# One attention and MoE kernel: where the next chunk's scores, k's transposition and the decays stand in the steady slots

## The chip, the cores and the metric

The kernel runs on one core of one Trainium2 chip. The metric is the device time of one execution in microseconds (us). The version before the change takes 626.73 us, the median of three executions (626.13 to 627.73).

## What is computed

Three stages follow each other, for 4 batches of 768 tokens with 384 channels (8 heads of 48). All arithmetic is fp32; a dense product is made of three products of a rounded part ("hi") and a rest ("lo").

```python
for t in range(S):                                   # stage 1
    state = alpha[:, :, t, :, None] * state + np.einsum('bhd,bhe->bhde', k[:, :, t], v[:, :, t])
    y[:, :, t] = np.einsum('bhd,bhde->bhe', q[:, :, t], state)
...
theta = x @ w_theta                                  # stage 2
zr = x * cos_t
zi = x * sin_t
y = w_tok_r @ zr + w_tok_i @ zi                      # mixes tokens
u = x + y
x2 = u + np.maximum(u @ w_ch, 0.0)
...
h = np.maximum(x2 @ w_in, 0.0)                       # stage 3: gate with a spatial mix
u, v = (h[..., :d_ff // 2], h[..., d_ff // 2:])
v_s = np.einsum('ts,bsd->btd', w_spatial, v_n) + b_spatial[None, :, None]
out = (u * v_s) @ w_out
```

## The kernel before

Stage 1 is done in chunks of 128 tokens: 6 chunks a batch, 24 in all (`ALL`), numbered g. Within a chunk the recurrence is turned into products: the decays are scanned (`decay_keys`, L738 and L742, and `decay_queries`, L747, on VectorE), keys and queries are multiplied by them (`scale_keys` L931, `scale_queries` L935, on GpSimd), the scores k times q are made on TensorE (`scores` L342), masked on VectorE (`mask_scores` L753), and multiplied by v, with the carried state's share added (`attend`, L370 and L375). The state is carried with a transposition of k (`turn_k` L332), its copy on ScalarE (`copy_kT` L552), the product with v (`keys_values` L354) and `update_state` (L769, L773) on VectorE. Each chunk's result x goes on at once to stage 2: copied (`copy_x` L557), transposed (`transpose_x` L382), split (`xT_high` L562, `xT_low` L780), kept (`keep_xT` L568), multiplied by w_theta (`angles` L391), reduced and put through sine and cosine (`whole_turns` L575 and L578, `reduce_angle` L786 to L792, `sines` L584 to L587), multiplied (`multiply_z` L797) and split again (`z_high` L598, `z_low` L948).

The program has a slot for each chunk. In the first six slots the kernel fills up. The 18 slots behind them, g = 6 to 23, are the steady ones: beside chunk g's stage 1 they hold stage 2 of the batch before. A steady slot has two units of `token_mix` (L409, 18 matmuls each; `ya` and `yb` in the code) and one tile of `channel_mix` (L428). A unit is one chunk of one half of a batch; six units fill the accumulator psY, and then `make_u` (L808, three instructions on VectorE) adds x and empties it. That is so in the slots with c = g % 6 equal to 0 and 3. The first unit of the next half follows in the next slot, and each third of it waits for its `make_u` (`u_made`). `make_x2` (L815) finishes a channel tile.

All engines run orders written out by hand, with semaphores between them; each executes its own list in that order. SyncE issues the transfers, in order too. `load_chunk(g)` brings decays, keys and queries of chunk g (L254, 770 KB, tile `akq`) and v (L255) into one of two buffers, and so waits until `attend(g-2)` has read the old contents. `store_x2` (L264) waits for `make_x2`, and stands in front of the load of chunk 2 of a batch (from the second steady batch on) and of that of chunk 5:

```python
for c in range(CHUNKS):
    load_chunk((b + 1) * CHUNKS + c)
    if c == 1 and b:
        store_x2(b - 1, 1)
    if c == 4:
        store_x2(b, 0)
```

The buffers of the partial sums in PSUM are psS (scores), psF (in two halves: psK for k's transposition and the state's product, psO for attention and x's transposition), psY and psC. Stage 3, behind the slots, is not touched by the change.

Of the kernel before, what the change touches and what calls it, by code (L numbers as in the profile page):

```python
# [24 lines left out]
CHUNKS = SEQ // P  # L25
# [11 lines left out]
ALL = BATCH * CHUNKS  # L37
LINKS = CHUNKS - 1
# [37 lines left out]
def build(nc, akq, v_in, w_theta, w_tok_rT, w_tok_iT, w_ch, w_in, w_spT, b_sp, w_out, out, x2_dram):  # L76
    ctx = ExitStack()
    with ctx:
# [246 lines left out]
        def _(pe):  # L325
            def turn_k(g):
                if g % CHUNKS == LINKS:
                    return
                pe.wait_ge(k_scaled, g + 1)
                need(pe, state_made, link(g))  # L330
                for p in range(PAIRS):
                    mm = pe.transpose(psK[:, tile(p)], K[g % 2][:, p, :], ident[:])  # L332
                mm.then_inc(kT_made, 1)

            def scores(g):
                s = g % 2
                pe.wait_ge(q_scaled, g + 1)
                need(pe, masked, g)
                for p in range(PAIRS):
                    for h in range(2):  # L340
                        rows = slice(64 * h, 64 * h + HD)
                        mm = pe.matmul(psS[:, h, p, :], K[s][rows, p, :], Q[s][rows, p, :],  # L342
                                       start=True, stop=True)
                mm.then_inc(scored, 1)
# [13 lines left out]
            def attend(g):  # L358
                s, c = g % 2, g % CHUNKS
                pe.wait_ge(v_arrived[s], 16 * (g // 2 + 1))  # L360
                pe.wait_ge(masked, g + 1)
                need(pe, xT_lo, g)
                need(pe, xT_kept, g)
                if c:
                    pe.wait_ge(state_made, link(g))
                for p in range(PAIRS):
                    for h in range(2):
                        e = slice(HD * (2 * p + h), HD * (2 * p + h + 1))
                        for rows in TOKEN_HALVES:
                            mm = pe.matmul(psO[rows, e], probs[:, h, p, rows], V[s][:, e],  # L370
                                           start=(p == 0 and h == 0), stop=False, skip_group_check=True)
                    if c:
                        pr = slice(2 * HD * p, 2 * HD * (p + 1))
                        for rows in TOKEN_HALVES:
                            mm = pe.matmul(psO[rows, pr], Q[s][:, p, rows], S[c % 2][:, p, :],  # L375
                                           start=False, stop=(p == PAIRS - 1), skip_group_check=True)
                mm.then_inc(attended, 1)

            def transpose_x(g):
                pe.wait_ge(x_copied, g + 1)  # L380
                for j in range(CT):
                    mm = pe.transpose(psO[:, tile(j)], x[g % 2][:, tile(j)], ident[:])  # L382
                mm.then_inc(xT_made, 1)
# [11 lines left out]
            def token_mix(unit):  # L395
                if unit is None:
                    return
                k, s = unit
                h = k % HALVES
                if k < HALVES:  # L400
                    pe.wait_ge(tok_lo, k * CHUNKS + s // 2 * 2 + 2)
                if h == 0:
                    pe.wait_ge(z_lo, k // HALVES * CHUNKS + s + 1)
                for j in range(CT):
                    if s == 0:
                        need(pe, u_made, (k - 1) * CT + j + 1)
                    for q, W in enumerate((WR, WI)):
                        for n, (l, m) in enumerate(PASSES):
                            mm = pe.matmul(psY[:, j, 0:HALF], Z[s][l][:, q, tile(j)], W[m][:, s, half(h)],  # L409
                                           start=(s == 0 and q == 0 and n == 0),  # L410
                                           stop=(s == CHUNKS - 1 and q == 1 and n == 2))
                    if s == CHUNKS - 1:
                        mm.then_inc(y_made, 1)
                if s < CHUNKS - 1:
                    mm.then_inc(mixed, 1)
# [17 lines left out]
            for c in range(CHUNKS):  # L433
                ya, yb = units(-1, c)
                turn_k(c)
                scores(c)
                if c == 1:
                    pe.wait_ge(theta_lo, 1)
                if c:
                    angles(c - 1, 0)  # L440
                token_mix(ya)
                keys_values(c)
                attend(c)
                transpose_x(c)
                token_mix(yb)
            angles(CHUNKS - 1, 0)
            for b in range(BATCH - 1):
                for c in range(CHUNKS):
                    g = (b + 1) * CHUNKS + c
                    ya, yb = units(b, c)  # L450
                    n = tile_of(b, c)
                    turn_k(g)
                    scores(g)
                    token_mix(ya)
                    keys_values(g)
                    attend(g)
                    channel_mix(n, g)
                    transpose_x(g)
                    token_mix(yb)
                    angles(g, 0 if n is None else n + 1)  # L460

# [51 lines left out]
            b = BATCH - 1  # L513
# [32 lines left out]
        def _(act):  # L546
            def copy_kT(g):
                if g % CHUNKS == LINKS:
                    return
                act.wait_ge(kT_made, link(g) + 1)  # L550
                need(act, kv_made, link(g))
                act.activation(kT[:].rearrange("p q d -> p (q d)"), psK, ACT.Copy).then_inc(kT_copied, 1)  # L552
# [75 lines left out]
            for c in range(CHUNKS):  # L628
# [13 lines left out]
                for i in SPLITS[c]:  # L642
                    tok_high(i)

            for b in range(BATCH - 1):
                for c in range(CHUNKS):
                    g = (b + 1) * CHUNKS + c
                    whole_turns(g - 1)
                    copy_kT(g)
                    if c == 1:  # L650
                        u_highs(HALVES * b)
                    if c == 4:
                        u_highs(HALVES * b + 1)
                    sines(g - 1)
                    z_high(g - 1)
                    copy_x(g)
                    xT_high(g)
                    keep_xT(g)
                    for i in SPLITS[g]:
                        tok_high(i)  # L660

# [66 lines left out]
        def _(dve):  # L728
# [93 lines left out]
            for c in range(CHUNKS):  # L822
                mask_scores(c)
                decay_keys(c + 1)
                if c:
                    reduce_angle(c - 1)
                decay_queries(c + 1)
                update_state(c)
                xT_low(c)
                if c:  # L830
                    multiply_z(c - 1)
            for b in range(BATCH - 1):
                for c in range(CHUNKS):
                    g = (b + 1) * CHUNKS + c
                    reduce_angle(g - 1)
                    mask_scores(g)
                    multiply_z(g - 1)
                    if g + 1 < ALL:
                        decay_keys(g + 1)
                        decay_queries(g + 1)  # L840
                    xT_low(g)
                    make_x2(tile_of(b, c))
                    update_state(g)
                    if c == 0:
                        make_u(HALVES * b)
                    if c == 3:
                        make_u(HALVES * b + 1)
# [79 lines left out]
        def _(pool):  # L927
# [42 lines left out]
            for c in range(CHUNKS):  # L970
                scale_keys(c + 1)
                scale_queries(c + 1)
                if c:
                    z_low(c - 1)
                if c == CHUNKS - 2:
                    pool.wait_ge(ch_hi, 1)
                    pool.tensor_tensor(WC[1][:], raw_ch[:], f(WC[0][:]), ALU.subtract).then_inc(ch_lo, 1)
                for i in SPLITS[c]:
                    tok_low(i)
            for b in range(BATCH - 1):  # L980
                for c in range(CHUNKS):
                    g = (b + 1) * CHUNKS + c
                    if c == 1:
                        u_lows(HALVES * b)
                    if c == 4:
                        u_lows(HALVES * b + 1)
                    z_low(g - 1)
                    if g + 1 < ALL:
                        scale_keys(g + 1)
                        scale_queries(g + 1)  # L990
                    for i in SPLITS[g]:
                        tok_low(i)
            z_low(ALL - 1)
# [68 lines left out]
```

## Time and profile before

| | |
|---|---|
| median of three executions | 626.73 us |
| the profiled execution: its own time | 626.28 us |
| the profiled execution: its span | 624.6 us |
| mean granted TensorE clock, share of full | 0.986 |
| TensorE busy with matmuls | 591.7 us, 95% |
| VectorE busy | 363.1 us, 58% |
| ScalarE busy | 224.0 us, 36% |
| GpSimd busy | 257.7 us, 41% |
| steady slots in the span | from about 81 us to 326 us |

The span is the time from the first to the last recorded instruction. A line such as `L409 PE MATMUL psY<-tok_r_hi,z_hi` names the line of the kernel, the engine (PE is TensorE's matmuls, PEld its weight loads, DVE VectorE, ACT ScalarE, POOL GpSimd, SPq the transfers that SyncE issues), the operation, and what it writes and reads. A float32 matmul counts twice in the profile, so that `scores`, 8 instructions in the program, appears as x16. In the chain of work that ended last, the start of a piece is the end of the piece before it.

### The profile page before, as it was taken

The page shows a single profiled execution, that of the slowest core. Times are in us where ns is not written, and L with a number is a line of the kernel's source. Part 1 is how long each engine was busy: PE and PEld are TensorE (multiplying, and loading weights), DVE is VectorE, ACT ScalarE, POOL GpSimd, SP SyncE. Part 2 cuts the span into 40 slices and gives each one's busy share as a digit, 9 for nine tenths or more (in the row PEclk, how much of TensorE's full clock was granted, in tenths as well). Part 3 has the DMA queues.
Part 4 walks back from the last instruction along what each step waited for, and adds up shares of the span by engine and source line. Part 5 has one row for each costly group of instructions (what it writes and reads, how often), then busy time and mean ns, then how long its engine had stood idle before and what let it go on. Part 6 is the DMA issues. An engine that isn't in the chain of part 4 may idle for free.

```text
span 624.6 us, 11166 instructions
## 1 busy us (share of the span) xinstructions
PE 591.7 (95%) x4608; PEld 560.6 (90%) x4608; DVE 363.1 (58%) x565; ACT 224.0 (36%) x410; POOL 257.7 (41%) x205
## 2 busy tenths in 40 slices
PE   4778989999999999999997999999999999999998
PEld 3667889999999999999996978998999899989997
DVE  5788666787786776877734037846333633373132
ACT  2544556343343444433434114623131313131210
POOL 5475578353463353644513017245313531352130
PEclk9978999999999999999998999999999999999999
DMA  8551321132141231320323073010220020002002
GB/s 314 203 178 65 111 82 64 64 102 66 65 165 65 61 106 65 105 95 32 102 102 114 0 266 114 8 70 2 76 77 2 0 77 1 0 1 77 0 2 77
DMA packets 20259, 49.54 MB, mean 79 GB/s; under 512 B 1648, under 2 KB 15216, under 8 KB 19696
## 3 DMA queue, kind: packets, MB, share of 16 engines
q1 hardware_dynamic: 20208, 48.81, 22.8%
q8 instruction: 37, 0.61, 0.4%
q14 instruction: 14, 0.11, 0.1%
HBM read 39.37 MB, written 9.44 MB: 78 GB/s over the span
## 4 chain that ended last, share of the span: by engine, by line
PE 86%; DVE 5%; ACT 3%; POOL 3%; issue 2%; DMA 0%; DVEq 0%; ACTq 0%; POOLq 0%
PE psY L409 22%; PE psF L508 8%; PE psS L508 8%; PE psC L391 7%; PE psC L428 7%; PE psS L486 5%; PE psS L342 5%; PE psF L476 5%; PE psF L486 3%; PE psS L496 3%; PE psF L496 3%; PE psF L370 3%; PE psS L476 3%; PE psF L375 2%; PE psF L332 2%
## 5 line engine op out<-in xcount | busy, mean ns | idle before, releaser
L948 POOL TENSOR_TENSOR z_lo<-cos_sin,z_hi 128x768 fp32r<-128x768 f32 x24 | 44.0, 1833 | 125.6 <-ACT z_hi L598 125.6
L1012 POOL TENSOR_TENSOR gated_lo<-u_gated,gated_hi 128x384 fp32r<-128x384 f32 x32 | 32.4, 1013 | 125.4 <-ACT gated_hi L698 125.3
L409 PE MATMUL psY<-tok_r_hi,z_hi 128*128 128x384 f32 x144 | 52.5, 365 | 4.7 <-POOL z_lo L948 4.3
L747 DVE TENSOR_TENSOR_SCAN akq<-akq,rtotal 128x516 f32<-128x516 f32 x24 | 54.7, 2281 | 0.7
L409 PE MATMUL psY<-tok_r_hi,z_lo 128*128 128x384 f32 x144 | 48.5, 337 | 0.0
L409 PE MATMUL psY<-tok_r_lo,z_hi 128*128 128x384 f32 x144 | 48.5, 337 | 0.0
L409 PE MATMUL psY<-tok_i_lo,z_hi 128*128 128x384 f32 x144 | 48.4, 336 | 0.0
L409 PE MATMUL psY<-tok_i_hi,z_lo 128*128 128x384 f32 x144 | 48.4, 336 | 0.0
L409 PE MATMUL psY<-tok_i_hi,z_hi 128*128 128x384 f32 x144 | 48.4, 336 | 0.0
L931 POOL TENSOR_TENSOR akq<-akq,after 128x512 f32<-128x512 f32 x24 | 44.7, 1862 | 4.9 <-DVE after L738 4.9
L698 ACT ACTIVATE gated_hi<-u_gated 128x384 fp32r<-128x384 f32 x32 | 16.8, 526 | 81.0 <-DVE u_gated L886 81.0
L955 POOL TENSOR_TENSOR u_lo<-u_f,u_hi 128x384 fp32r<-128x384 f32 x24 | 24.4, 1046 | 50.2 <-ACT u_hi L603 50.2
L786 DVE SCALAR_TENSOR_TENSOR psC<-turns,psC 128x384 f32<-128x384 f32 x24 | 13.5, 562 | 53.3 <-ACT turns L578 53.2
L370 PE MATMUL psF<-v,scores 128*64 128x48 f32 x768 | 36.7, 223 | 0.5 <-DVE scores L753 0.5
L738 DVE TENSOR_TENSOR_SCAN after<-akq,restart 128x516 f32<-128x516 f32 x24 | 33.7, 1403 | 3.6 <-DMA akq<-akq 3.6
L753 DVE TENSOR_TENSOR scores<-psS,mask 128x1024 f32<-128x1024 f32 x24 | 29.2, 1217 | 11.2 <-PE psS L342 11.2
L1006 POOL TENSOR_TENSOR vn_lo<-vt,vn_hi 128x512 fp32r<-128x512 f32 x24 | 31.2, 1305 | 8.4 <-ACT vn_hi L683 8.4
L409 PEld LDWEIGHTS psY<-tok_r_hi,z_hi 128*128 128x128 f32 x144 | 27.3, 189 | 7.7 <-POOL z_lo L948 3.6
L575 ACT ACTIVATE turns<-psC 128x384 f32<-128x384 f32 x24 | 11.8, 490 | 62.0 <-PE psC L391 62.0
L370 PEld LDWEIGHTS psF<-v,scores 128*64 128x64 f32 x768 | 31.8, 141 | 1.6 <-issue 1.6
L508 PE MATMUL psF<-sp_hi,vn_hi 128*128 128x384 f32 x96 | 32.2, 335 | 0.8 <-DVE sp_lo L913 0.8
L935 POOL TENSOR_TENSOR akq<-akq 128x512 f32<-128x512 f32 x24 | 28.5, 1186 | 10.4 <-DVE akq L747 10.4
(141 smaller groups left out, 1747.3 us busy)
## 6 DMA issues: line engine op xcount, KB each, us to landing
akq<-akq SPq DMA_DIRECT2D x23, 770.0 KB, 4.5
v<-v_in SPq DMA_DIRECT2D x24, 192.0 KB, 4.7
x_dram<-u_f SPq DMA_DIRECT2D x8, 576.0 KB, 3.7
x_raw<-x_dram SPq DMA_DIRECT2D x4, 1152.0 KB, 5.5
out<-ot SPq DMA_DIRECT2D x24, 192.0 KB, 1.9
raw_tok_r<-w_tok_rT SPq DMA_DIRECT2D x6, 384.0 KB, 7.8
raw_tok_i<-w_tok_iT SPq DMA_DIRECT2D x6, 384.0 KB, 8.7
raw_sp<-w_spT SPq DMA_DIRECT2D x1, 2304.0 KB, 8.9
```

The costliest lines, as they stand in the source:

```text
L370: mm = pe.matmul(psO[rows, e], probs[:, h, p, rows], V[s][:, e], start=(p == 0 and h == 0), stop=False, skip_group_check=True)
L391: mm = pe.matmul(psC[:, 0:D], XT[g % 2][l][:, j, :], WT[m][:, j, :], start=(j == 0 and k == 0), stop=(j == CT - 1 and k == 2))
L409: mm = pe.matmul(psY[:, j, 0:HALF], Z[s][l][:, q, tile(j)], W[m][:, s, half(h)], start=(s == 0 and q == 0 and n == 0), stop=(s == CHUNKS - ...
L428: mm = pe.matmul(psC[:, 0:HALF], WC[l][:, j, tile(m_out)], U[m][:, j, :], start=(j == 0 and k == 0), stop=(j == CT - 1 and k == 2))
L476: mm = pe.matmul(banks[n % RING], X2[l][:, j, tile(i)], WN[m][:, j, G:FF], start=(j == 0 and k == 0), stop=(j == CT - 1 and k == 2))
L486: mm = pe.matmul(banks[n % RING][:, 0:D], GA[l][:, j, tile(i)], WO[m][:, j, :], start=(j == 0 and k == 0), stop=(j == GT - 1 and k == 2))
L496: mm = pe.matmul(banks[n % RING][:, 0:HALF], WN[l][:, j, tile(j_out)], X2[m][:, j, half(h)], start=(j == 0 and k == 0), stop=(j == CT - 1 ...
L508: mm = pe.matmul(banks[n % RING][:, 0:HALF], VN[l][:, s, tile(j)], WS[m][:, s, half(h)], start=(s == 0 and k == 0), stop=(s == CHUNKS - 1 ...
L738: dve.tensor_tensor_scan(after[:, ::-1], ALPHA[s][:, ::-1], restart[:, ::-1], 1.0, ALU.mult, ALU.add).then_inc(after_made, 1)
L747: dve.tensor_tensor_scan(ALPHA[s], ALPHA[s], rtotal[:, 1:], rtotal[:, 0:1], ALU.mult, ALU.add).then_inc(decayed, 1)
L931: pool.tensor_tensor(K[g % 2], K[g % 2], AFTER[:, :, 1:SEG], ALU.mult).then_inc(k_scaled, 1)
L948: pool.tensor_tensor(Z[c][1][:], trigs[g % 2][:], f(Z[c][0][:]), ALU.subtract).then_inc(z_lo, 1)
```

## The change

In the steady slots TensorE makes the scores of chunk g+1 right behind the attention of chunk g, where those of chunk g stood at the head of the slot, and transposes k of chunk g+1 right behind x of chunk g. The first two (for g = 6) are put into the last filling slot. On VectorE the state's update and the mask of chunk g+1 come earlier, and the decays, now those of chunk g+2, stand behind `xT_low` and ahead of `make_u`; decays for chunk 7 stand ahead of the steady slots. GpSimd scales chunk g+2, and ScalarE copies k's transposition at the end of a slot. SyncE's list stays.

```diff
 # TensorE
                 attend(c)
+                if c == LINKS:
+                    scores(CHUNKS)
                 transpose_x(c)
+                if c == LINKS:
+                    turn_k(CHUNKS)
                 token_mix(yb)
...
-                    turn_k(g)
-                    scores(g)
                     token_mix(ya)
                     keys_values(g)
                     attend(g)
+                    if g + 1 < ALL:
+                        scores(g + 1)
                     channel_mix(n, g)
                     transpose_x(g)
+                    if g + 1 < ALL:
+                        turn_k(g + 1)
                     token_mix(yb)
 # ScalarE
+            copy_kT(CHUNKS)
...
                     whole_turns(g - 1)
-                    copy_kT(g)
...
                     keep_xT(g)
+                    if g + 1 < ALL:
+                        copy_kT(g + 1)
 # VectorE
+            mask_scores(CHUNKS)
+            decay_keys(CHUNKS + 1)
+            decay_queries(CHUNKS + 1)
...
                     reduce_angle(g - 1)
-                    mask_scores(g)
                     multiply_z(g - 1)
+                    update_state(g)
                     if g + 1 < ALL:
-                        decay_keys(g + 1)
-                        decay_queries(g + 1)
+                        mask_scores(g + 1)
+                    make_x2(tile_of(b, c))
                     xT_low(g)
-                    make_x2(tile_of(b, c))
-                    update_state(g)
+                    if g + 2 < ALL:
+                        decay_keys(g + 2)
+                        decay_queries(g + 2)
                     if c == 0:
                         make_u(HALVES * b)
                     if c == 3:
                         make_u(HALVES * b + 1)
 # GpSimd
+            scale_keys(CHUNKS + 1)
+            scale_queries(CHUNKS + 1)
...
                     z_low(g - 1)
-                    if g + 1 < ALL:
-                        scale_keys(g + 1)
-                        scale_queries(g + 1)
+                    if g + 2 < ALL:
+                        scale_keys(g + 2)
+                        scale_queries(g + 2)
                     for i in SPLITS[g]:
                         tok_low(i)
```

How the rows move is shown at two places. The first is VectorE's list in slot g = 9 (c = 3 of the first steady batch). The scans are printed under the operation they are built from; L738 and L747 are the two of the decays, u_f_0_82<-psC is `make_x2`, and u_f_1_83<-psY is `make_u`. Before:

```order
L753 TENSOR_TENSOR scores<-psS,mask 128x1024
L797 TENSOR_TENSOR cos_sin_97<-x_73,cos_sin_97 128x768
L738 SCALAR_TENSOR_TENSOR after<-akq_86,restart 128x516
L742 RECIPROCAL rtotal<-after 128x4
L747 SCALAR_TENSOR_TENSOR akq_86<-akq_86,rtotal 128x516
L780 TENSOR_TENSOR xT_lo<-psF,xT_hi 128x384
L815 SCALAR_TENSOR_TENSOR u_f_0_82<-psC,u_f_0_82 128x384
L769 TENSOR_TENSOR psF<-psF,state_94 64x192 x2
L773 TENSOR_TENSOR state_93<-psF,after 64x4x48 x2
L808 TENSOR_TENSOR u_f_1_83<-psY,xT_kept_80 128x384 x3
```

And after the change, with new line numbers (each is 8 higher):

```order
L805 TENSOR_TENSOR cos_sin_97<-x_73,cos_sin_97 128x768
L777 TENSOR_TENSOR psF<-psF,state_94 64x192 x2
L781 TENSOR_TENSOR state_93<-psF,after 64x4x48 x2
L761 TENSOR_TENSOR scores<-psS,mask 128x1024
L823 SCALAR_TENSOR_TENSOR u_f_0_82<-psC,u_f_0_82 128x384
L788 TENSOR_TENSOR xT_lo<-psF,xT_hi 128x384
L746 SCALAR_TENSOR_TENSOR after<-akq_87,restart 128x516
L750 RECIPROCAL rtotal<-after 128x4
L755 SCALAR_TENSOR_TENSOR akq_87<-akq_87,rtotal 128x516
L816 TENSOR_TENSOR u_f_1_83<-psY,xT_kept_80 128x384 x3
```

The decays moved from ahead of `xT_low` to the place directly in front of `make_u`, and they read the other buffer, akq_87: that of chunk 11, which slot 9's own attention (chunk 9) has to leave first.

The second place is TensorE's list from chunk 6 on, in the last filling slot, as the difference between the two programs:

```order
 L370 MATMUL psF<-v_90,scores 64x48 x4
 L375 MATMUL psF<-state_94,akq_87 64x96 x2
+L342 MATMUL psS<-akq_86 128x128 x8
 L382 MATMUL psF<-ident,x_74 128x128 x3
-L409 MATMUL psY<-tok_r_hi,z_hi 128x384
...
 L332 MATMUL psF<-ident,akq_86 128x128 x4
-L342 MATMUL psS<-akq_86 128x128 x8
+L409 MATMUL psY<-tok_r_hi,z_hi 128x384
```

Scores stand behind attention now, and k's transposition behind that of x; the token mix and the angles follow. In the steady slots the two go the same way, one slot ahead of their chunk.

## Rows read from the trace of the kernel before

**Rows 1.** Waits of TensorE over the span: waited for, us, times, longest

```profile
PE psY L409 <- POOL z_lo L948: 4.3, 2, 3.3
...
PE psY L409 <- DVE u_f L808: 0.4, 1, 0.4
```

**Rows 2.** Chain of waits, slot 15: start us, us, what

```profile
203.80 1.09 PE psS L342 x16
204.89 3.35 PE psY L409 x18
208.24 0.60 PE psF L354 x16
...
210.45 1.78 PE psC L428 x9
...
212.56 3.12 PE psY L409 x18
215.68 1.56 PE psC L391 x9
...
218.77 3.34 PE psY L409 x18
```

**Rows 3.** Timeline of VectorE, slot 15: start us, us, what

```profile
208.46 1.23 DVE L738 TENSOR_TENSOR_SCAN after<-akq,restart 128x516 f32<-128x516 f32 x1
...
209.94 2.48 DVE L747 TENSOR_TENSOR_SCAN akq<-akq,rtotal 128x516 f32<-128x516 f32 x1
...
213.59 0.55 DVE L815 SCALAR_TENSOR_TENSOR u_f<-psC,u_f 128x384 f32<-128x384 f32 x1
...
215.59 1.49 DVE L808 TENSOR_TENSOR u_f<-psY,xT_kept 128x384 f32<-128x384 f32 x3
```

**Rows 4.** Timeline of the transfers that SyncE issues, slots 15 and 16

```profile
214.17 0.53 SPq L264 DMA_DIRECT2D x_dram<-u_f  x1
214.74 0.62 SPq L254 DMA_DIRECT2D akq<-akq  x1
```

**Rows 5.** Landing of loads L254: that of slot 15, of slot 18, then the page, all 23

```profile
L254 SPq DMA_DIRECT2D akq<-akq x1: 617/617/617, 214.7 to 214.7; - x1
DMA to landing us min/median/max: 5.7/5.7/5.7
L254 SPq DMA_DIRECT2D akq<-akq x1: 617/617/617, 254.8 to 254.8; - x1
DMA to landing us min/median/max: 6.6/6.6/6.6
...
akq<-akq SPq DMA_DIRECT2D x23, 770.0 KB, 4.5
```

**Rows 6.** Timeline, VectorE scan L747 in the second filling slot

```profile
13.89 2.10 DVE L747 TENSOR_TENSOR_SCAN akq<-akq,rtotal 128x516 f32<-128x516 f32 x1
```

**Rows 7.** Timeline of GpSimd at the same place: keys scaled

```profile
13.72 1.18 POOL L931 TENSOR_TENSOR akq<-akq,after 128x512 f32<-128x512 f32 x1 [1.17 <-DVE after L738]
```

**Rows 8.** Chain of waits, slot 18 (c = 0)

```profile
250.49 1.76 PE psC L428 x9
...
258.80 3.35 PE psY L409 x18
```

**Rows 9.** Windows: us, busy PE, PEld, DVE, ACT, POOL, PEclk, DMA share, GB/s

```profile
36.80:40.70 3.90, 0.00 (x0) 0.00 (x0) 3.81 (x7) 1.82 (x4) 2.54 (x3) 0.88 0.62 238
40.80:46.50 5.70, 5.70 (x28) 5.15 (x29) 3.86 (x4) 2.55 (x4) 3.44 (x2) 0.50 0.00 0
...
330.50:333.70 3.20, 0.00 (x0) 0.00 (x0) 0.90 (x2) 0.84 (x1) 1.80 (x1) 0.93 0.55 141
333.70:336.60 2.90, 2.86 (x9) 2.86 (x10) 1.73 (x2) 2.82 (x3) 0.00 (x0) 0.50 0.94 290
```

**Rows 10.** Timeline of GpSimd before the first steady slot

```profile
75.49 1.20 POOL L935 TENSOR_TENSOR akq<-akq 128x512 f32<-128x512 f32 x1 [1.17 <-DVE akq L747]
```

**Rows 11.** Timeline of TensorE at the same place: transposition of x of chunk 5

```profile
75.25 0.44 PE L382 MATMUL psF<-ident,x 128*128 128x128 f32 x2 [0.59 <-ACT x L557]
```

## The prediction

> **What bounds the kernel now.** I read four views in this order. First the waits of TensorE: in the steady slots almost nothing is there. A token mix waited for `z_low` twice, 4.3 us in all, and for `make_u` once, 0.4 us [rows 1]. So in these slots the span is TensorE's own work, one instruction behind another, and the chain of waits says the same: in slot 15 each piece is TensorE's, and from one first token mix to the next it takes 218.77 - 204.89 = 13.88 us [rows 2]. Whatever the other engines do there is hidden as long as it comes in time. Second, the same chain prices the order of TensorE's pieces. Third, VectorE's timeline shows what its list holds in front of `make_u`, which the next half's token mix needs. Fourth, the transfers: where in SyncE's list the loads stand and when they land.
>
> **TensorE's own pieces.** Nothing is added or taken away, only moved. Eighteen matmuls of the token mix take 3.12 us when they follow other full-size matmuls, and 3.35 when they follow the scores, whose operands have 48 rows [rows 2]. Nine take 1.56 us as angles and 1.78 as the channel tile behind attention, whose outputs have 64 columns. So it costs about 0.2 us to come to full size from a small form. Before, a slot pays that twice, behind the scores and behind attention; after, scores follow attention directly, and full size is entered once. The token mix gets back 3.35 - 3.12 = 0.23 us. The scores' own entry stays in their 1.09 us if it costs the same from attention as from a transposition. No row shows that entry. It could be free, or cost two entries; by 0.2 us either way the gain of a slot is 0 to 0.45. I take 0.23, since both known entries are that size. The Trainium skill (TensorEngine Tiling (Array Packing), Key Properties) states that a change of the tiling mode drains the engine, and not a change of tile within one. No run here shows attention followed by scores. By that rule every slot has three changes instead of four, and the gain is one entry a slot, as I take it. From the first token mix of slot 7 to that of slot 23 there are 16 slots: **-3.7 us** (0 to -7).
>
> **The decays, and what they stand in front of.** `decay_keys(g+2)` in slot g needs the load of chunk g+2. That goes into the buffer that `attend(g)` reads, so it cannot start before slot g's attention has ended. In a plain slot this is in time: the median load lands 4.5 us after issue [rows 5], about when `xT_low` is through, and VectorE's next work is due only when the angles end.
>
> In five slots it isn't: g = 9, 12, 15, 18 and 21. There SyncE's list has a `store_x2` in front of the load, which waits for that slot's `make_x2`. In slot 15 `make_x2` ends at 213.59 + 0.55, the store is issued at 214.17 and the load at 214.74 [rows 3, 4]. It lands 5.7 us later, and in slot 18 even 6.6 [rows 5]. Before, nobody minded: that chunk was wanted a slot later. Now VectorE stops for it, in order, and behind the decays, in the same five slots, stands `make_u`. The first token mix of the next slot waits for `make_u`, and it now stands right behind the angles; the k transposition and scores that used to stand between are gone.
>
> Slot 15 by its rows, with the first token mix at 204.89 as before. Attention ends 0.23 earlier, at 210.45 - 0.23 = 210.22; scores until 211.31 (1.09); channel tile until 213.09 (1.78) [rows 2]. `make_x2` takes 0.55 more, and ends at about 213.7 with the hand-over; the load is issued 0.57 us behind the store, at 214.3, and lands at 220.0. Then the first scan and the reciprocal, 209.94 - 208.46 = 1.48 [rows 3]; and the second scan. That took 2.48 us in slot 15, where GpSimd worked beside it on two jobs, and 2.10 where GpSimd only scaled the keys [rows 6, 7], which is the order here: 2.10. Then the first third of `make_u`, 1.49 / 3 = 0.5, and 0.05 for the hand-over: 224.15. TensorE would be ready for the token mix at 218.77 - 0.23 = 218.54. **It waits 5.6 us.** I take that for slots 9, 15 and 21. For slot 18 the channel tile starts at 250.49 and the next first mix at 258.80 [rows 8]: channel ends at 250.49 - 0.23 + 1.09 + 1.78 = 253.13, load issued at 254.3, landed after 6.6 at 260.9, mix possible at 265.0 against 258.57: 6.4 us. For slot 12 the same with some 5.9 for the landing: 5.8. Together 3 x 5.6 + 6.4 + 5.8 = **+29.0 us**. Bounds: each landing between 4.5 and 6.6 gives 23 to 33.
>
> **The clock.** A wait of this length was followed by half rate: after 3.2 us without a matmul the granted clock was 0.50 for 2.9 us, and after 3.9 us for 5.7 us (1.2 instead of 2.4 GHz) [rows 9]. Nine matmuls took those 2.9 us, 0.32 each, against 3.12 / 18 = 0.173 [rows 2], so 46% of such a stretch is lost: 1.3 us and 2.6 us. I take 2.0 for each of the five waits: **+10 us** (0 to 15; the upper end is a stretch somewhat longer than the longer one). The Trainium skill (TensorE: Matmul & The Clock Gate, Why this matters for your kernels) warns of exactly such idle gaps between bursts of matmuls, since the array falls back to half rate; the trace agrees in these two places, with 0.50.
>
> **The seam.** The scores of chunk 6 now stand in the last filling slot, behind the attention of chunk 5, which ended at 75.25 - 0.59 = 74.66 [rows 11]. Their queries are scaled only at 75.49 + 1.20 = 76.69 [rows 10]. TensorE waits 2.0 us instead of 0.6, and x of chunk 5, its sines and `z_low` move back with it. Then `scale_keys(7)` and `scale_queries(7)` stand on GpSimd behind two splits of token weights and ahead of `z_low(5)`, for which the mix already waits [rows 1]; and slot 6 also has decays in front of `make_u`, here with a load that isn't held up. I take **+2.8**: 1.4 for the first wait and as much again for the second. Bounds 0 and 6.
>
> **Hidden, at nothing.** `copy_kT` one place earlier on ScalarE, which idles over half of each slot. `update_state` now comes well before `turn_k` of the next chunk overwrites its half of psF. `make_x2` ahead of `xT_low`: both wait for TensorE. In the slots behind the five waits everything moves by the same amount; the sines come later against attention, but x is copied with about half a microsecond to spare.
>
> **Sum.** 626.3 (the profiled execution's own time; the median is 0.4 higher) - 3.7 + 29.0 + 10 + 2.8 = 664.4, so **664 us**.
>
> **Rivals.**
> - *The waits come, the clock holds.* Five waits of 6 us, but no half rate behind them: 654 us. For it: only two gaps of the trace bear on it. Against: both fell. Chance 0.13.
> - *The delay runs on.* After a late `make_u` angles are reduced late, so the sines and ScalarE's copy of x come late, and the half microsecond of room is gone: 1 to 3 us more for each of five, 674 us. Chance 0.12.
> - *The load isn't held by the store.* If it left with the end of attention and landed in 4.5 us, slot 15 would give 210.22 + 0.1 + 4.5 + 1.48 + 2.10 + 0.55 = 218.95 against 218.54, 0.4 us too late in each of six slots with `make_u`: 626.3 - 3.7 + 2.8 + 2.5 = 628 us. Against: the loads at 214.74 and 254.8 left only behind the store. Chance 0.03.
> - *Faster.* The decays come in time everywhere, and the merged small forms give their 3.7 us: 622.6 us. It decides on one point: the first third of `make_u` must be done when the angles end, and even with no store in front of the load it would be 0.4 us late by the working above. What speaks for it is that TensorE waits nowhere in these slots now. Chance 0.03.
>
> **How the numbers follow.** The forecast has 0.69, the rivals 0.13, 0.12, 0.03 and 0.03. The range leaves out the last two and a part of the tails: low is the first rival with the smaller landings and the larger gain, 652; high is the second rival with the larger landings, 678. A measurement of this kernel can tell about 0.3% from no change, 1.9 us. Faster by more: 0.03. Within it: 0.02. Slower by more: 0.95.
>
> **What would show it.** Right: in the waits of TensorE, `L409 <- make_u` with five entries of 5 to 7 us, and VectorE's first scan waiting for the load five times; the granted clock at 0.50 behind most of them; in plain slots a period of 13.65 us, the first token mix at 3.12, and the scores still 1.09. Scores at 0.9 or 1.3 would show my entry price wrong. A wait for `make_u` that is short, or a load that lands before `xT_low` in these five slots, would make the whole prediction wrong.

## The result and the profile after

The changed kernel takes 668.83 us, the median of four executions (665.40 to 671.02), against 626.43 us (625.32 to 627.73): a ratio of 1.067 (ratios here are of the means), 95% interval 1.062 to 1.072. It is slower by 42 us. The forecast was 664 us, in a range of 652 to 678.

| | before | after |
|---|---|---|
| the profiled execution: own time, span | 626.28, 624.6 us | 671.02, 669.3 us |
| mean granted TensorE clock | 0.986 | 0.952 |
| TensorE busy | 591.7 us | 605.8 us |
| VectorE busy | 363.1 us | 363.3 us |

The waits of TensorE after, where the columns are the us in total, times and longest, answer to [rows 1]. The line numbers of VectorE are 8 higher than before; those of GpSimd are 12 higher:

```profile
PE psY L409 <- DVE u_f L816: 27.8, 6, 5.5
...
PE psS L342 <- POOL akq L947: 5.4, 3, 2.2
PE psY L409 <- POOL z_lo L960: 3.3, 1, 3.3
```

The wait of the token mix for `make_u` went from one of 0.4 us to six with 27.8 us; the one of 0.4 is still there, behind the slots. What `make_u` stood behind is in the chain of waits, from slot 9's channel tile to the first mix of slot 10 (start us, us, what). It answers to slot 15 in [rows 2 to 4]:

```profile
136.50 1.80 PE psC L428 x9
...
138.32 0.57 DVE u_f L823
...
138.91 0.61 SPq L264
...
139.56 5.50 DMA akq<-akq
...
145.08 1.25 DVE after L746
...
146.56 0.03 DVE akq L755
146.60 1.98 issue
148.58 0.54 DVE u_f L816
149.12 0.14 issue
149.26 0.98 PE psY L409 x2
```

Read it from above. The channel tile releases `make_x2`; that releases x2's store; behind the store leaves the load of chunk 11. 5.50 us later it lands, the first scan starts, then the reciprocal, then the second scan. That scan stands in this chain as 0.03 and "issue" 1.98; in VectorE's timeline it takes 2.10 us, with GpSimd's scaling of the keys beside it (146.39 to 147.57), where the shortest of its 24 scans took 1.28. Then comes the first third of `make_u`, and only then the mix. In slot 9 the angles ended at 143.76, 5.50 us ahead of that mix. The clock over the idle stretch and behind it is in the windows view (us, busy time of PE, PEld, DVE, ACT, POOL, granted clock, DMA share, GB/s), for two of the five waits:

```profile
143.80:149.20 5.40, 0.00 (x0) 0.00 (x0) 4.05 (x5) 1.07 (x3) 1.64 (x2) 0.81 0.21 84
149.30:154.00 4.70, 4.70 (x15) 4.70 (x16) 3.04 (x6) 2.76 (x6) 3.65 (x4) 0.50 0.00 0
...
240.40:245.70 5.30, 0.00 (x0) 0.00 (x0) 4.05 (x5) 1.00 (x3) 1.64 (x2) 0.72 0.17 67
245.80:249.50 3.70, 3.70 (x12) 3.70 (x13) 2.67 (x5) 2.19 (x5) 3.63 (x4) 0.50 0.00 0
```

In the 4.7 us behind the first wait there are 15 matmuls of 0.31 us each, where full rate needs 0.173. A plain slot, that of chunk 8, reads in the chain of waits:

```profile
116.38 3.12 PE psY L409 x18
119.51 0.60 PE psF L354 x16
...
121.72 1.09 PE psS L342 x16
122.81 1.79 PE psC L428 x9
124.60 0.33 PE psF L382 x3
124.93 0.44 PE psF L332 x4
125.36 3.15 PE psY L409 x18
128.51 1.56 PE psC L391 x9
130.07 3.12 PE psY L409 x18
```

From 116.38 to 130.07 it takes 13.69 us, against 13.88 in [rows 2]: the first mix is at 3.12 instead of 3.35, the scores still at 1.09, the channel tile at 1.79. So the merged small forms do bring something, 0.2 us a slot.

**Where the 44.7 us between the two spans are.** The first mix of slot 7 and that of slot 23 start, in the timeline of TensorE before, at

```profile
95.39 0.44 PE L409 MATMUL psY<-tok_r_hi,z_hi 128*128 128x384 f32 x1
...
313.81 0.45 PE L409 MATMUL psY<-tok_r_hi,z_hi 128*128 128x384 f32 x1
```

and after, at

```profile
102.53 0.33 PE L409 MATMUL psY<-tok_r_hi,z_hi 128*128 128x384 f32 x1
...
356.52 0.33 PE L409 MATMUL psY<-tok_r_hi,z_hi 128*128 128x384 f32 x1
```

The 16 slots between grew from 218.42 to 253.99 us, by 35.6. What stands ahead of them grew by 7.1 us, of which 0.7 was there before the first changed instruction; what stands behind, by 2.0 us.

### The profile page after: what moved, and what is told of

The parts are those of the page before. It is cut to its first block, busy times and chain, and to the rows that moved or that the text cites. A ratio compares the mean times of both kernels' runs of the same rounds, so it can differ in the third digit from the quotient of the medians.

```text
span 669.3 us, 11166 instructions
## 1 busy us (share of the span) xinstructions
PE 605.8 (91%) x4608; PEld 576.5 (86%) x4608; DVE 363.3 (54%) x565; ACT 223.8 (33%) x410; POOL 245.3 (37%) x205
## 4 chain that ended last, share of the span: by engine, by line
PE 75%; DVE 9%; DMA 6%; issue 3%; POOL 3%; ACT 2%; SPq 0%; DVEq 0%; ACTq 0%
PE psY L409 19%; PE psS L514 7%; PE psF L514 7%; PE psC L428 5%; PE psS L342 5%; DMA akq<-akq 5%; PE psS L492 4%; PE psC L391 4%; PE psF L482 4%; PE psF L502 4%; PE psS L502 3%; PE psF L492 3%; PE psF L370 2%; DVE after L746 2%; DMA bias<-b_sp 2%
## 5 line engine op out<-in xcount | busy, mean ns | idle before, releaser
L409 PE MATMUL psY<-tok_r_hi,z_hi 128*128 128x384 f32 x144 | 54.9, 381 | 31.1 <-DVE u_f L816 27.8
L943 POOL TENSOR_TENSOR akq<-akq,after 128x512 f32<-128x512 f32 x24 | 29.7, 1237 | 87.6 <-DVE after L746 86.1
L409 PEld LDWEIGHTS psY<-tok_r_hi,z_hi 128*128 128x128 f32 x144 | 29.7, 206 | 33.5 <-issue 17.4
L746 DVE TENSOR_TENSOR_SCAN after<-akq,restart 128x516 f32<-128x516 f32 x24 | 37.0, 1540 | 33.1 <-DMA akq<-akq 32.7
L409 PE MATMUL psY<-tok_r_lo,z_hi 128*128 128x384 f32 x144 | 51.8, 360 | 0.0
L409 PE MATMUL psY<-tok_r_hi,z_lo 128*128 128x384 f32 x144 | 51.3, 356 | 0.0
L755 DVE TENSOR_TENSOR_SCAN akq<-akq,rtotal 128x516 f32<-128x516 f32 x24 | 49.4, 2058 | 0.7
L805 DVE TENSOR_TENSOR cos_sin<-x,cos_sin 128x768 f32<-128x768 f32 x24 | 23.7, 986 | 31.3 <-ACT cos_sin L593 31.3
L342 PE MATMUL psS<-akq 48*128 48x128 f32 x384 | 32.5, 316 | 5.4 <-POOL akq L947 5.4
L342 PEld LDWEIGHTS psS<-akq 48*128 48x128 f32 x384 | 27.4, 216 | 9.3 <-POOL akq L947 6.2
```

The lines of the kernel that those rows point to most:

```text
L746: dve.tensor_tensor_scan(after[:, ::-1], ALPHA[s][:, ::-1], restart[:, ::-1], 1.0, ALU.mult, ALU.add).then_inc(after_made, 1)
L755: dve.tensor_tensor_scan(ALPHA[s], ALPHA[s], rtotal[:, 1:], rtotal[:, 0:1], ALU.mult, ALU.add).then_inc(decayed, 1)
```

## Experiments

The theory has three parts. VectorE stops at a scan that wants a load which the store holds up, and `make_u` is queued behind the scan. TensorE falls to half rate over the wait. And the seam costs something of its own. Each run but the fourth starts from the changed kernel.

**Only `make_u` back ahead of the decays.**

```diff
+                    if c == 0:
+                        make_u(HALVES * b)
+                    if c == 3:
+                        make_u(HALVES * b + 1)
                     if g + 2 < ALL:
                         decay_keys(g + 2)
                         decay_queries(g + 2)
-                    if c == 0:
-                        make_u(HALVES * b)
-                    if c == 3:
-                        make_u(HALVES * b + 1)
```

> The changed kernel with make_u ahead of the decays again in VectorE's list; the load still leaves behind the store of x2. Theory (VectorE stands at the scan that wants the load, and make_u is queued behind it): the five waits of the token mix for make_u, 27.4 us, and the half rate behind them, 10.1 us, go. But the late decays then hold the next slot: the queries of chunk g+2 are scaled about 1.7 us after the scores want them, and x's transposition waits about 1.3 us for a copy that stands behind late sines. Some 3 us in each of five slots stay: about 646 us. Rival A (only the place of make_u matters, the late load costs nothing by itself): 631 us. Rival B (the wait has another cause): 668 us.

Measured: 664.29 us, one execution. A miss by 18 us, in the direction of rival B; but the wait did move. TensorE's waits:

```profile
PE psC L428 <- POOL u_lo L967: 12.4, 6, 2.6
PE psS L342 <- POOL akq L947: 11.1, 8, 2.8
...
PE psY L409 <- DVE u_f L816: 0.2, 1, 0.2
```

The wait for `make_u` is gone, and two others took its place: the channel tile's for the splits of u, and the scores' for their queries. The timeline of GpSimd in slot 16 tells why the first of them is so long:

```profile
244.42 1.18 POOL L943 TENSOR_TENSOR akq<-akq,after 128x512 f32<-128x512 f32 x1 [8.42 <-DVE after L746]
246.77 1.18 POOL L947 TENSOR_TENSOR akq<-akq 128x512 f32<-128x512 f32 x1 [1.17 <-DVE akq L755]
247.90 3.84 POOL L967 TENSOR_TENSOR u_lo<-u_f,u_hi 128x384 fp32r<-128x384 f32 x3
```

GpSimd stands 8.42 us at the keys that wait for the late scan, and the splits of u, for which the channel tile waits, are queued behind. I had followed VectorE's and ScalarE's lists and left out GpSimd's. The slots behind the five late loads (10, 13, 16, 19 and 22) took 4.5 to 6.8 us more than plain slots of their kind, 26.9 us in all where 15 were expected: the late load costs by itself, also where it blocks GpSimd's list and not `make_u`. In each of them two waits close behind each other, of 0.8 to 1.4 us and of 1.8 to 2.65 us, were followed by half rate. The rest of the miss has nothing to do with the store. Slot 7 took 20.85 us, against 13.69 in the changed kernel, since its channel tile waited 4.74 us: in slot 6 the decays of chunk 8 now stand behind `make_u`, and GpSimd's splits of u behind them and 4.5 us of token weights.

**Only the store behind the load.**

```diff
-                    if c == 1 and b:
+                    if c == 2 and b:
                         store_x2(b - 1, 1)
-                    if c == 4:
+                    if c == 5:
                         store_x2(b, 0)
```

> The changed kernel with each store of x2 one place later in SyncE's list, behind the load that it held up; VectorE's order as changed. Theory: the load leaves with the end of attention and lands 4.2 to 4.5 us later, as in the plain slots; the decays end about 0.4 us too late for make_u in six slots. The five long waits and the half rate go: 668.8 - 27.4 - 10.1 + 2.4 = 634 us. Rival (the load is late because x2's store and the load share the transfer engines, whatever the order): landings stay near 5.5 us, still 4 us earlier than now, five waits of about 1.5 us: 640 us.

Measured: 632.91 us, median of four (631.53 to 633.22), ratio to the kernel before 1.010 (1.008 to 1.012). The theory's 634 holds. The load of chunk 17 left with the end of attention, 5.5 us into slot 15 instead of 9.6, in the timeline of SyncE's transfers and in the view of that load, which landed after 4.0 us instead of 5.6:

```profile
215.97 0.33 SPq L254 DMA_DIRECT2D akq<-akq  x1
...
DMA to landing us min/median/max: 4.0/4.0/4.0
```

The other four took 4.1 to 4.2 us, so the rival is out. There is no half rate from slot 8 to the end of the slots. What is left of the wait for `make_u` is seen in the periods alone: slot 9 takes 13.92 us where a plain slot takes 13.69, 0.2 us for the 0.4 expected. (TensorE's list of waits has one of 1.8 us for `make_u`; it lies behind the slots, in the run-out.)

From the first mix of slot 7 (101.68) to that of slot 23 (318.83) it takes 217.15 us, 1.3 less than before. So the stores in front of five loads account for 36 of the 42 us. The rest is the seam, 6.4 us here too (32.13 us from the last filling slot's first mix to slot 7's, 25.76 before), less what the slots gain.

**Useless matmuls in the wait.**

```diff
                     angles(g, 0 if n is None else n + 1)
+                    if c == 3 or (c == 0 and b):
+                        pe.wait_ge(masked, g + 2)
+                        for _ in range(28):
+                            pe.matmul(psS[:, 0].rearrange("p q t -> p (q t)")[:, 0:HALF], WT[0][:, 0, 0:P],
+                                      WR[0][:, 0, 0:HALF], start=True, stop=True)
```

> The changed kernel with 28 full-size matmuls (4.85 us at full rate) of no use put behind the angles in the five slots whose next token mix waits; they write to a part of the score sums that nobody reads. Theory (the array falls to half rate because it is idle for 5.5 us): the clock stays at full rate in these slots, the waits in the trace shrink to about 0.6 us, and the 10.1 us of half rate come back: about 659 us. Rival (the half rate has another cause, or its cost is hidden): 668 us.

Measured: 663.22 us, one execution. The clock did what the theory says, here before and behind two of the waits:

```profile
138.00:149.70 11.70, 10.78 (x65) 10.42 (x63) 5.22 (x8) 2.50 (x6) 1.81 (x3) 1.00 0.44 135
149.90:154.00 4.10, 4.10 (x46) 3.85 (x48) 2.63 (x5) 2.54 (x6) 3.61 (x4) 1.00 0.02 4
285.00:290.20 5.20, 4.57 (x27) 4.25 (x25) 3.90 (x5) 0.77 (x2) 1.49 (x2) 1.00 0.17 62
290.40:296.00 5.60, 5.60 (x84) 5.23 (x86) 3.97 (x7) 3.02 (x7) 3.71 (x4) 1.00 0.00 0
```

From the first mix behind each wait to the first mix of the next slot it took 13.3, 15.4, 13.3, 13.8 and 13.3 us, in place of 15.5, 16.1, 15.1, 15.9 and 15.0: 8.5 us less. The second of them kept part of its half rate: there the load took 7.2 us to land instead of 5.7, and the matmuls ran out 2.1 us ahead of `make_u` (0.8 to 1.0 us in the other four slots). That slot explains most of the 4 us above the 659 expected: 1.6 us of half rate that stayed, and 1.5 us of a later `make_u`. The rest is 0.7 us in slot 7, where the channel tile waited, and 0.1 to 0.4 us in each of the other four. The half rate comes from the idle array, and cost 1.7 to 2.2 us in each of the four waits where it went.

**The kernel before with the store behind the load**, the edit of the stores on the old kernel.

> The kernel before with the store of x2 behind the load, nothing else. Theory: nobody waits for these loads there, so nothing changes: 626 us. Rival (the early load or the later store has a price or a gain of its own): another time by over 2 us.

Measured: 623.6 us, one execution; the kernel before showed 623.13 to 627.87 in the same session. From the first mix of slot 6 to that of slot 23 this took 231.84 us, against 231.86 in the kernel before: nothing changed where the edit is. The 2.4 us lie ahead of it, in the filling slots, where half rate fell on 7.8 us of TensorE's work in place of 12.6; 46% of the difference is 2.2 us. With executions of the kernel before between 623.13 and 627.87, one time alone can't tell 2 us; the slots in the trace can.

**`make_u` between the two scans**, with the store behind the load.

```diff
                     if g + 2 < ALL:
                         decay_keys(g + 2)
-                        decay_queries(g + 2)
                     if c == 0:
                         make_u(HALVES * b)
                     if c == 3:
                         make_u(HALVES * b + 1)
+                    if g + 2 < ALL:
+                        decay_queries(g + 2)
```

> The kernel with the stores behind the loads (632.9 us) and, besides, make_u between the two scans of the decays: behind decay_keys, ahead of decay_queries. Theory: what is left of the wait for make_u is the second scan's 2.1 us in front of it; without it the six slots lose nothing there, and their periods fall to the plain slots' 13.68 us (13.0 where c is 0): 1.8 us less, about 631 us. Rival (the later second scan holds the next slot's sines or queries instead): no gain, 633 us or more.

Measured: 634.17 us, median of four (633.23 to 635.18): the rival's number, but not for its reason. From slot 8 on the slots went as the theory has them: first mixes at 120.06, 133.75 and 147.44, 13.69 apart, slot 9 among them, and 201.6 us from slot 8 to slot 23 against 203.2 with the store alone moved. Slots 6 and 7 ate the gain. In slot 6 the scores waited 2.8 us for their queries, no longer than with the store alone moved (2.7), but half rate behind that wait lasted 6.8 us instead of 3.4, and the slot took 18.1 us instead of 16.9; why it lasted longer, no run here tells. Slot 7 took 16.2 us instead of 14.0, since its channel tile waited 2.5 us: GpSimd's splits of u stand behind its scaling of the queries of chunk 8 (104.35 to 105.54), and that behind the second scan, which comes later now. That is the seam again, made longer.

**Token weights behind the scaling of chunk 7**, with the store behind the load.

```diff
-                for i in SPLITS[c]:
+                for i in SPLITS[c] if c < LINKS else ():
                     tok_low(i)
             scale_keys(CHUNKS + 1)
             scale_queries(CHUNKS + 1)
+            for i in SPLITS[LINKS]:
+                tok_low(i)
```

> The kernel with the stores behind the loads (632.9 us) and, besides, the two splits of token weights of the last filling slot behind the scaling of chunk 7 in GpSimd's list. Theory (at the seam the scores of chunk 7 wait for GpSimd, which works off 5.5 us of token weights first): the second wait of the scores, about 2.2 us, and the half rate behind it go; the first one, for the queries of chunk 6, stays: about 630 us. Rival (the seam waits for the sines of chunk 5 anyway): the wait moves to z_low, 633 us.

Measured: 634.44 us, one execution. The rival's time came, and a wait did move, though not to `z_low` in the main. Idle times ahead of TensorE's instructions at the seam, from its timeline:

```profile
76.35 1.85 PE L342 MATMUL psS<-akq 48*128 48x128 f32 x16 [2.07 <-POOL akq L947]
84.88 0.41 PE L409 MATMUL psY<-tok_r_hi,z_hi 128*128 128x384 f32 x1 [0.17 <-POOL z_lo L960]
93.49 0.75 PE L382 MATMUL psF<-ident,x 128*128 128x128 f32 x3 [2.59 <-ACT x L563]
95.78 0.66 PE L409 MATMUL psY<-tok_r_hi,z_hi 128*128 128x384 f32 x1 [0.68 <-POOL z_lo L960]
```

The scores of chunk 7 no longer wait, and the transposition of x waits instead, 2.59 us, for a copy that stands behind sines which are late since the first wait. Half rate behind it lasted 6.8 us. The seam is one chain; taking its second link away moves the wait.

**The scores behind the transpositions**, on the kernel with `make_u` between the scans, with the mask behind `xT_low`.

```diff
                     attend(g)
-                    if g + 1 < ALL:
-                        scores(g + 1)
                     channel_mix(n, g)
                     transpose_x(g)
                     if g + 1 < ALL:
                         turn_k(g + 1)
+                        scores(g + 1)
                     token_mix(yb)
```

> The kernel of e_between with the scores of chunk g+1 not behind attention but behind the transpositions of x and k, so that small forms and full size alternate as before the change; the mask goes behind xT_low for it. Theory (coming back to full size costs 0.2 us and the changed order saves one such entry): a plain slot takes 13.88 us again instead of 13.68, 3 us more over 16 slots, 634 us. Rival (the gain of a slot came from somewhere else, k's transposition beside x's for instance): the period stays at 13.68.

Measured: 644.68 us, one execution. The total says little, because slots 5 to 7 lost some 5 us more (in slot 6 a wait of 4.3 us for x's copy, in slot 7 one of 3.5 us of the channel tile, each with half rate behind it). The slots say it:

```profile
193.70 3.12 PE psY L409 x18
...
201.15 0.44 PE psF L332 x4
201.58 1.09 PE psS L342 x16
202.67 3.32 PE psY L409 x18
206.00 1.56 PE psC L391 x9
207.56 3.12 PE psY L409 x18
```

13.86 us a slot instead of 13.69, with the 0.2 us now in the mix that follows the scores. The gain of the change is the full-size entry that it saves; k's transposition beside x's, which this run keeps, brings 0.02 us at most (13.88 before).

**The new order begun a slot later**, on the kernel with `make_u` between the scans.

```diff
 # TensorE
+                    if g < CHUNKS + 2:
+                        turn_k(g)
+                        scores(g)
                     token_mix(ya)
                     keys_values(g)
                     attend(g)
-                    if g + 1 < ALL:
+                    if CHUNKS < g < ALL - 1:
                         scores(g + 1)
 # VectorE
                     reduce_angle(g - 1)
+                    if g < CHUNKS + 2:
+                        mask_scores(g)
                     multiply_z(g - 1)
+                    if g == CHUNKS:
+                        decay_keys(g + 1)
+                        decay_queries(g + 1)
                     update_state(g)
```

and nothing of chunks 6 and 7 ahead of the steady slots (the diff shows the main places); `turn_k`, `copy_kT`, `mask_scores` and GpSimd's scaling follow suit.

> The kernel of e_between with the new order begun one slot later: slot 6 in the old order, the new one from slot 7 on, where the decays of chunk 8 come at the end of slot 6, behind the first steady mix. Theory (the seam cost 6.4 us because scores were pulled into a place where their queries were not yet scaled): the seam costs nothing, the first mix of slot 7 starts at about 95.4 us as in the kernel before, and 16 slots bring 0.2 us each: 626.4 - 3.2 = 623.5 us, faster than the kernel before by 0.5%. Rival (some lead must be paid wherever the order changes): slot 6 or 7 grows by 2 us or more, and nothing is won: 626 us.

Measured: 625.67 us, median of twelve, against 627.13: ratio of the means 0.9995 (0.998 to 1.001). No difference, the rival's number. The seam's 6.4 us were gone, and the slots from 8 on each brought 0.2 us. But slot 7 took 15.4 us, since its channel tile waited 1.6 us: on GpSimd the splits of u ended only at 104.4, behind 5.2 us of token weights and the scaling of chunk 8.

**The same with that wait taken away**: in slot 6 `make_u` ahead of both decays, and on GpSimd two splits of token weights one slot later.

```diff
 # VectorE
+                    if g == CHUNKS:
+                        make_u(0)
                     if g + 2 < ALL:
                         decay_keys(g + 2)
-                    if c == 0:
+                    if c == 0 and b:
                         make_u(HALVES * b)
 # GpSimd
                         scale_keys(g + 1)
                         scale_queries(g + 1)
+                    if g == CHUNKS + 1:
-                        for i in SPLITS[g]:
+                        for i in SPLITS[CHUNKS]:
                             tok_low(i)
```

> The kernel of e_late_between with two places changed at the seam: in slot 6 make_u stands ahead of both decays of chunk 8, and two splits of token weights on GpSimd come one slot later, so that the splits of u are no longer queued behind 5 us of them. Theory (e_late_between won its 0.2 us in each slot, and lost 1.7 us in slot 7 because the channel tile waited for GpSimd's u_low): slot 7 shrinks by that, and the kernel takes about 624 us against 627.1 for the kernel before, faster by 0.3 to 0.5%. Rival (slot 7 then waits for the sines or queries of chunk 8, which come later now): 625.7 us again.

Measured: 624.02 us, median of eleven (623.22 to 626.73), against 626.78: ratio 0.9962, 95% interval 0.9947 to 0.9978. The first mixes of slot 7 and slot 23:

```profile
93.88 0.44 PE L409 MATMUL psY<-tok_r_hi,z_hi 128*128 128x384 f32 x1
...
309.46 0.33 PE L409 MATMUL psY<-tok_r_hi,z_hi 128*128 128x384 f32 x1
```

215.58 us, against 218.42: 2.8 us less. This version beats both kernels, by 0.4% and, across two sessions, by 6.7%.

## Why the prediction was right

- **What bounds the kernel**: right. TensorE's own work fills a plain slot, before and after.
- **TensorE's pieces**, -3.7 us forecast: 13.88 - 13.69 = 0.19 a slot, about 3.0 over 16. The entry of the scores from attention cost just what I took (1.09 us for the scores, again). The 0.03 us that are missing went to the second mix (3.15 instead of 3.12). The scores put back between full-size pieces bring the 0.2 us back, so this is shown.
- **The five waits**, +29.0 us forecast: 5.50, 5.46, 5.47, 5.54 and 5.37 us, 27.3 together. The places, the order of events and the 2.10 us of the second scan came as worked out; the loads of slots 12 and 18 landed after 5.7 us each, instead of 5.9 and 6.6. Two slips in the working change nothing: by its own numbers slot 12 gives 5.7 us, not 5.8, and the bounds are 22 to 32, not 23 to 33.
- **The clock**, +10 us: half rate lasted 4.8, 5.2, 3.8, 4.6 and 3.6 us into the work behind the five waits, 22.0 us; 46% of it is 10.1. With matmuls in the waits 8.5 us of it came back, and one wait kept a part.
- **The seam**, +2.8 us forecast, bounds 0 and 6: 6.4 us, counted from the last filling slot's first mix (25.76 us to slot 7's before, 32.20 after). This is the term that was mis-sized. The first wait was where I put it, 2.07 us. The second was not: I had the mix wait for `z_low(5)`, and it is the scores of chunk 7 that wait, 2.22 us, for the queries that GpSimd scales behind the token weights. The waits alone grew by less than I took: 4.3 us, against 2.2 in the same places before (0.59, 0.59 and 0.98). What I left out is that each was followed by half rate: 3.4 us of it from 78.9 on and 6.8 from 92.6 on, by the 46% 4.7 us. In the latter 16 scores took 2.08 us instead of 1.09 and the mix 4.63 instead of 3.12. I had charged the clock to the long waits alone, though the trace of the kernel before shows short ones with half rate behind them (the last section has them).
- **Hidden, at nothing**: right for `copy_kT`, `update_state` and `make_x2`. None of them shows up among the waits of TensorE in the steady slots behind the seam.
- **The rivals**: the clock didn't hold, and the delay didn't run on into the slots behind. The rival with an unheld load, 628 us, was built: 632.9 us. Of the 5 us in between 3.6 are the seam; the rest is that this kernel's median lies 1.4 us above its profiled execution, 631.53. Its counterpart on the fast side exists, 624.0, but needs, besides the stores behind the loads, `make_u` between the scans, a later beginning and the two edits at the seam.
- **The sum**: in the 16 slots -3.7 + 29.0 + 10 = 35.3 us were forecast and 35.6 measured. That is closer than the terms deserve, and in part luck: the three as measured make 34.4, and each wait cost some 0.16 us beyond its length, which I hadn't thought of (slot 9: 19.35 - 5.50 = 13.85, against 13.69). The profiled execution, 671.02, lies 6.6 us above the forecast: 3.6 are the seam's, and 0.7 and 2.0 stand ahead of the changed instructions and behind the slots, where nothing was forecast.

## What to carry to other kernels

Before moving an operation ahead by half a slot, find the buffer that its input goes into and the last reader of that buffer: that sets the earliest time, and whatever the load's own queue has in front of it comes on top. Then look at what stands behind the moved operation on its engine, on every engine that waits for it: here `make_u` on VectorE, and the splits of u on GpSimd as soon as `make_u` was out of the way. And begin a new order where its inputs exist, not at the first place where the loop allows it; a gain of 0.2 us a slot needs 30 slots to pay for a seam of 6 us.

## What was not expected of the hardware

Short waits were enough for half rate. In the changed kernel 2.07 us without a matmul, up to 77.4, and 2.22 us, up to 92.7, were each followed by it; the windows view, with the columns as above, shows the two stretches behind them:

```profile
78.90:82.30 3.40, 3.40 (x14) 3.40 (x13) 1.83 (x3) 2.49 (x6) 0.00 (x0) 0.50 0.20 74
92.70:99.30 6.60, 6.60 (x32) 6.09 (x33) 5.61 (x8) 4.16 (x7) 3.00 (x2) 0.50 0.29 115
```

At 46% lost, these cost up to 1.6 and 3.1 us. The kernel before shows the same in its filling slots: 2.06 us without a matmul, up to 28.33 and up to 52.30, and half rate for 3.4 us behind each. From its timeline of TensorE and its windows:

```profile
28.33 0.63 PE L332 MATMUL psF<-ident,akq 128*128 128x128 f32 x4 [2.06 <-DVE state L773]
...
29.50:32.90 3.40, 3.40 (x18) 3.18 (x17) 2.55 (x3) 2.79 (x4) 2.31 (x2) 0.50 1.00 363
...
53.40:56.80 3.40, 3.40 (x19) 3.18 (x16) 2.49 (x3) 2.06 (x3) 2.24 (x2) 0.50 0.02 5
```

The length of a wait doesn't settle it. With `make_u` between the scans a wait of 2.48 us in slot 7 (110.47 to 112.95) had no half rate behind it. And the same wait of 3.31 us behind the slots was followed by 3.4 us of half rate in the kernel before, by 6.8 with `make_u` between the scans, and by none with the store alone moved. So a wait of 2 us at TensorE is better counted as 3 to 5 us in a plan, and a single execution can come out without it.

The other surprise is the load that took 7.2 us to land where all others behind a store took 5.5 to 6.6; why, no run here tells.
